# Adding the causal mask of batches 1 to 3 on GpSimd, to per-tile decay rows, instead of by a matmul into the scores

## The reference, cut to what matters

```python
def _attn_ref(q, k, v, f) -> np.ndarray:
    scores = scale * np.matmul(q, k.transpose(0, 1, 3, 2))
    log_f = np.log(np.clip(f, 0.0001, 1.0))
    cum = np.cumsum(log_f, axis=-1)
    decay = cum[:, :, :, None] - cum[:, :, None, :]
    causal = np.triu(np.ones((S, S), dtype=bool), k=1)
    scores = np.where(causal, -1000000000.0, scores + decay)
    scores = scores - np.max(scores, axis=-1, keepdims=True)
    attn = np.exp(scores)
    attn = attn / (np.sum(attn, axis=-1, keepdims=True) + 1e-09)
    return np.matmul(attn, v).astype(np.float32)
```

## Time and profile before

| what | value |
|---|---|
| median of 3 runs | 764.41 us (762.1 to 766.06) |
| the profiled execution's own time | 765.94 us |
| its span in the profile | 764.2 us |
| TensorE busy | 717.7 us (94%) |
| VectorE busy | 444.7 us (58%) |
| ScalarE busy | 437.0 us (57%) |
| GpSimd busy | 399.3 us (52%) |
| data moved | 96.65 MB, 126 GB/s over the span |

### The profile page before, as it was taken

How to read it: one execution, slowest core, us unless ns; L and a number is a source line. 1 busy time by engine, 2 the same in 40 slices (tenths; PEclk the granted TensorE clock), 3 DMA queues, 4 the chain that set the end, 5 groups by cost and what they waited for, 6 DMA issues and landing times.

```text
span 764.2 us, 15776 instructions
## 1 busy us (share of the span) xinstructions
PE 717.7 (94%) x6027; PEld 681.0 (89%) x6027; DVE 444.7 (58%) x1255; ACT 437.0 (57%) x1031; POOL 399.3 (52%) x439
## 2 busy tenths in 40 slices
PE   3999979999999999999999999999999999998993
PEld 3888879999999999999999989999999999995562
DVE  5898957676776646675656466766542332224323
ACT  4788866575757675666576665757554344311113
POOL 4355357474747764565657564848385476520000
PEclk9999989999999999999999999999999999998897
DMA  4433323332333333333331413332214454598976
GB/s 104 106 92 106 94 65 89 87 94 81 95 94 96 95 94 81 87 105 91 100 91 51 126 28 95 94 108 67 69 43 141 135 169 163 161 401 348 357 307 247
DMA packets 90362, 96.65 MB, mean 126 GB/s; under 512 B 61296, under 2 KB 61296, under 8 KB 88240
## 3 DMA queue, kind: packets, MB, share of 16 engines
q1 hardware_dynamic: 90288, 95.66, 40.6%
HBM read 90.84 MB, written 4.79 MB: 125 GB/s over the span
## 4 chain that ended last, share of the span: by engine, by line
PE 79%; DVE 10%; ACT 7%; issue 2%; DMA 0%; POOL 0%; SPq 0%; DVEq 0%; POOLq 0%
PE mb L1204 51%; PE yb L1057 6%; PE zb L1076 6%; PE xb L1103 5%; PE mb L1256 2%; DVE prob L838 2%; PE xb L1037 2%; ACT prob L689 2%; PE yb L1295 1%; ACT xh L713 1%; DVE ptl L844 1%; PE yb L1059 1%; DVE kl L806 1%; DVE qs L802 1%; ACT qs L681 1%
## 5 line engine op out<-in xcount | busy, mean ns | idle before, releaser
L1204 PE MATMUL mb<-xh,wih 128*128 128x288 f32 x512 | 159.1, 311 | 7.8 <-DVE xl L855 4.3
L1204 PE MATMUL mb<-gh,woh 128*128 128x288 f32 x512 | 156.5, 306 | 3.5 <-DVE x2t L932 3.5
L1204 PE MATMUL mb<-xl,wih 128*128 128x288 f32 x512 | 151.6, 296 | 0.0
L1204 PE MATMUL mb<-xh,wil 128*128 128x288 f32 x512 | 151.6, 296 | 0.0
L1204 PE MATMUL mb<-gl,woh 128*128 128x288 f32 x512 | 150.8, 294 | 0.0
L1204 PE MATMUL mb<-gh,wol 128*128 128x288 f32 x512 | 150.8, 294 | 0.0
L643 POOL TENSOR_TENSOR gl<-hid,gh 128x288 fp32r<-128x288 f32 x128 | 105.0, 825 | 74.9 <-ACT gh L730 73.3
L925 DVE SCALAR_TENSOR_TENSOR hid<-gate,mb 128x288 f32<-128x288 f32 x128 | 57.7, 451 | 116.0 <-ACT gate L736 114.9
L689 ACT ACTIVATE prob<-prob,m_row 64x576 f32<-64x576 f32 (+4 forms) x160 | 96.4, 604 | 35.3 <-DVE m_row L824 34.4
L660 POOL TENSOR_TENSOR wol<-stage,woh 128x512 fp32r<-128x512 f32 x64 | 82.9, 1295 | 62.0 <-ACT woh L675 62.0
L660 POOL TENSOR_TENSOR wil<-stage,wih 128x512 fp32r<-128x512 f32 x64 | 82.1, 1290 | 57.0 <-ACT wih L675 56.9
(11 more groups left out here) (196 smaller groups left out, 1471.1 us busy)
## 6 DMA issues: line engine op xcount, KB each, us to landing
stage<-in_moe_w_in SPq DMA_DIRECT2D x64, 256.0 KB, 3.0
stage<-in_moe_w_out SPq DMA_DIRECT2D x64, 256.0 KB, 2.6
ring_a<-in_moe_w SPq DMA_DIRECT2D x16, 1024.0 KB, 6.9
ring_b<-in_moe_w SPq DMA_DIRECT2D x14, 1024.0 KB, 11.8
cum_b<-cum_dram SPq DMA_DIRECT2D x32, 288.0 KB, 3.7
qk_in<-in_q SPq DMA_DIRECT2D x32, 144.0 KB, 3.0
qk_in<-in_k SPq DMA_DIRECT2D x32, 144.0 KB, 3.5
v_in<-in_v SPq DMA_DIRECT2D x32, 128.0 KB, 3.2
```

The lines of the kernel that those rows point to most:

```text
L1204: ins = mm(bank[:, 0:HALF], a[:, t, P * (j % 4):P * (j % 4) + P], x[:, t, cols], start=(i == 0), stop=(i == 11))
```

## The change

For batches 1 to 3 the mask matmul is left out. The decay row is no longer one row of 576 columns for all tiles, but one piece for each tile, `cum_t[parity]`, at the columns `COFF[i]`: tile 3 at 0, tile 0 at 512, tile 2 at 640, tile 1 at 1024 and tile 4 at 1280, 1856 columns in all. For odd heads it lies in the enlarged `cum_1`, for even heads in the part of `x2tok` that belongs to batch 2. SP loads tile 4's piece where it loaded the row before, and the other four behind the slot's loads of v, q and k. GpSimd adds the mask to the diagonal blocks of these pieces: tile 4's in a step `cmask_4` right behind dup (64x64), the others in a step `cmask` at the place of the next head's first score group near the slot's end, in two additions of two blocks each (tiles 3 and 2, then tiles 0 and 1). VectorE waits for these instead of for the load. Batch 0 stays as it was.

```diff
@@ -40,6 +40,8 @@
 QW = [128, 128, 128, 128, 64]
 POFF = [0, 128, 384, 768, 1280]
 PW = 1920
+CW = 1856
+COFF = [512, 1024, 640, 0, 1280]
 PT_ALL = 1600
 KOFF = [0, 576, 1024, 1344, 1536]
 QK_AT = 224
@@ -186,7 +188,8 @@
         dup = following_head("dup")
         early = following_head("score")
         if engine == "pool":
-            qk, dup = qk + dup, []
+            qk, dup = qk + dup + following_head("cmask_4"), []
+            early = following_head("cmask")
         norm = at(scoring, "norm", s)
         vsplit = at(scoring and engine == "pool", "vsplit", s)
         pv_first, pv = at(before, "pv_first", s - 1), at(before, "pv", s - 1)
@@ -290,7 +293,9 @@
         mask_r = sb("mask_r", [P, P], F32R, att_mem)
         qk_in = sb("qk_in", [LD, 2, NLD, 2, DIM], F32, att_mem)
         v_in = sb("v_in", [P, 2, QT, DIM], F32, att_mem)
-        cum_b = sb("cum_b", [P, 2, SEQ], F32, att_mem)
+        cum_1 = sb("cum_1", [P, CW], F32, att_mem)
+        cum_b = cum_1[:, 0:2 * SEQ].rearrange("p (x n) -> p x n", x=2)
+        cum_t = (x2tok[:, 2 * QT:3 * QT, :].rearrange("p i n -> p (i n)")[:, 0:CW], cum_1[:, :])
         qs = sb("qs", [P, 2, QT * P], F32R, att_mem)
         kh = sb("kh", [P, 2, SEQ], F32R, att_mem)
         kl = sb("kl", [P, 2, SEQ], F32R, att_mem)
@@ -370,6 +375,9 @@
         qk_dma = [sem(f"qk_dma{i}") for i in range(2)]
         v_dma = [sem(f"v_dma{i}") for i in range(2)]
         c_dma = [sem(f"c_dma{i}") for i in range(2)]
+        c_dma_4 = [sem(f"c_dma_4{i}") for i in range(2)]
+        c_masked = sem("c_masked")
+        c_masked_4 = sem("c_masked_4")
         w_dma = [sem(f"w_dma{i}") for i in range(2)]
         e_dma = [sem(f"e_dma{i}") for i in range(NR)]
         out_dma = sem("out_dma")
@@ -462,6 +470,10 @@
                 return last_tokens[i] if kind == "token" else yb[:, 0, :] if kind == "logits" else zb[:, 0, :]
             return mb[:, place[kind, m, i] % 2, :]
 
+        def cum_loaded(n):
+
+            return 16 * (n // 2 + 1) if n < HEADS else 64 + 16 * (QT - 1) * (n // 2 - 3)
+
         def is_last(m):
             return isinstance(m, int) and m == BATCH - 1
 
@@ -526,8 +538,20 @@
             def load_cum(b, s):
                 n = b * 8 + s
                 wait_from(sp, decayed, 5 * (n - 1))
-                src = cum_dram[bass.ds(n, 1), :].to_broadcast([P, SEQ])
-                sp.dma_start(cum_b[:, s % 2, :], src).then_inc(c_dma[s % 2], 16)
+                if n < HEADS:
+                    sp.dma_start(cum_b[:, s % 2, :], cum_dram[bass.ds(n, 1), :].to_broadcast([P, SEQ])
+                                 ).then_inc(c_dma[s % 2], 16)
+                    return
+                sp.dma_start(cum_t[s % 2][0:QW[4], COFF[4]:CW], cum_dram[bass.ds(n, 1), :].to_broadcast([QW[4], SEQ])
+                             ).then_inc(c_dma_4[s % 2], 16)
+
+            def load_cum_tiles(b, s):
+
+                n = b * 8 + s
+                for i in (3, 2, 0, 1) if n >= HEADS else ():
+                    w = P * i + QW[i]
+                    sp.dma_start(cum_t[s % 2][:, COFF[i]:COFF[i] + w], cum_dram[bass.ds(n, 1), 0:w].to_broadcast([P, w])
+                                 ).then_inc(c_dma[s % 2], 16)
 
             def step(b, m, st):
                 if st[0] == "load":
@@ -536,6 +560,7 @@
                     n = b * HEADS + st[1]
                     if 0 < n < BATCH * HEADS - 1:
                         load_qk((n + 1) // HEADS, (n + 1) % HEADS)
+                    load_cum_tiles(b, st[1])
                 elif st[0] == "weights":
                     load_w(st[1], st[1] // 4, st[1] % 4, 0)
                 elif st[0] == "unit":
@@ -616,6 +641,20 @@
                     pool.wait_ge(k_lo, n + 1)
                     pool.tensor_tensor(kl[64:P, par, :], kl[0:64, par, :].bitcast(F32), zero, ALU.add).then_inc(k_dup, 1)
                     pool.wait_ge(k_dup, 2 * n + 2)
+                elif st[0] == "cmask_4":
+                    n = b * 8 + st[1]
+                    if n >= HEADS:
+                        pool.wait_ge(c_dma_4[n % 2], 16 * (n // 2 - 3))
+                        at = cum_t[n % 2][0:QW[4], COFF[4] + 4 * P:CW]
+                        pool.tensor_tensor(at, at, mask[0:QW[4], 0:QW[4]], ALU.add).then_inc(c_masked_4, 1)
+                elif st[0] == "cmask":
+                    n = b * 8 + st[1]
+                    if n >= HEADS:
+                        pool.wait_ge(c_dma[n % 2], cum_loaded(n))
+                        blocks = cum_t[n % 2][:, P * 3:P * 10].rearrange("p (x n) -> p x n", n=P)
+                        for at in (blocks[:, 0:5:4, :], blocks[:, 1:7:5, :]):
+                            pool.tensor_tensor(at, at, mask[:, :].unsqueeze(1).broadcast_to([P, 2, P]), ALU.add
+                                               ).then_inc(c_masked, 1)
                 elif st[0] == "vsplit":
                     s = st[1]
                     n = b * 8 + s
@@ -815,14 +854,20 @@
                     if g == 0:
                         if s == 0 and isinstance(b, int) and b == 0:
                             dve.wait_ge(cum_out, 16)
-                        dve.wait_ge(c_dma[par], b * 64 + 16 * (s // 2 + 1))
+                        if b:
+                            dve.wait_ge(c_masked_4, b * 8 + s - HEADS + 1)
+                        else:
+                            dve.wait_ge(c_dma[par], cum_loaded(s))
                         wait_from(dve, p_tr, b * 32 + 4 * (s - 1))
+                    elif g < 3 and b:
+                        dve.wait_ge(c_masked, 2 * (b * 8 + s - HEADS) + g)
                     nc.vector.memset(carrier[:, g:g + 1], 0.0)
                     for i in SCORE_ORDER[g]:
                         r, w = QW[i], P * i + QW[i]
                         base, o = SCORE_AT[i], POFF[i]
+                        decay = cum_t[par][0:r, COFF[i]:COFF[i] + w] if b else cum_b[0:r, par, 0:w]
                         nc.vector.tensor_tensor_reduce(
-                            prob[0:r, par, o:o + w], ybf[0:r, base:base + w], cum_b[0:r, par, 0:w], 1.0, 3e38,
+                            prob[0:r, par, o:o + w], ybf[0:r, base:base + w], decay, 1.0, 3e38,
                             ALU.add, ALU.min, m_row[0:r, par, i:i + 1]).then_inc(decayed, 1)
                 elif st[0] == "norm":
                     s, par = st[1], st[1] % 2
@@ -1054,10 +1099,11 @@
                         base = SCORE_AT[i]
                         for k0, kw in ((0, HALF), (HALF, HALF)) if i == 4 else ((0, w),):
                             for x, last in ((kh, False), (kl, True)):
-                                mm(ybf[:, base + k0:base + k0 + kw], qs[:, par, P * i:P * i + P],
-                                   x[:, par, k0:k0 + kw], start=not last, stop=last, skip_group_check=True)
-                        ins = mm(ybf[:, base + P * i:base + P * i + r], ident_r[:, :], mask_r[:, 0:r],
-                                 start=False, stop=True, skip_group_check=True)
+                                ins = mm(ybf[:, base + k0:base + k0 + kw], qs[:, par, P * i:P * i + P],
+                                         x[:, par, k0:k0 + kw], start=not last, stop=last, skip_group_check=True)
+                        if b == 0:
+                            ins = mm(ybf[:, base + P * i:base + P * i + r], ident_r[:, :], mask_r[:, 0:r],
+                                     start=False, stop=True, skip_group_check=True)
                     ins.then_inc(scored, 1)
                 elif st[0] == "pt":
                     s, c = st[1], st[2]
```

## The result

The changed kernel takes 775.6 us in the median (773.9 to 777.6, 4 runs) beside 763.25 for the kernel before (4 runs): a ratio of 1.015, 95% interval 1.012 to 1.018. It is slower by 12 us where 9.2 were to be gained. Its profiled execution took 773.85 us, with a span of 772.1.

The account below looks back on a forecast made before the run. TensorE was taken as the bound in batches 1 to 3. From the profiled 765.94 us, - 13.0 + 2.0 + 1.8 gave 756.7; from the runs' median, 764.4 - 9.2 gave 755.2 us, with an 8-in-10 range of 750 to 761.

Parts of the forecast that it names:

- TensorE bounds batches 1 to 3, so a matmul less is time less: In batches 1 to 3 TensorE is always busy, so each instruction removed saves time if no other engine comes late.
- 13.0 us for 120 matmuls: On TensorE in batches 1 to 3, each removed mask matmul saves one weight load's spacing, 0.108 us; range 7 to 26.
- GpSimd gets 1.9 us a head: GpSimd's three mask additions per head take 0.36 and twice 0.76 us, 45 us over 24 heads, fitting its idle time.
- Waits for weight splits 0, for masked rows 0: GpSimd's additions make neither TensorE wait for weight splits (smallest distance 2.4 us) nor VectorE for masked rows: cost 0.
- The shared work of VectorE and GpSimd, 2.0 us in the MLP stages with a bound of 8: GpSimd's additions lengthen VectorE's normalising multiplies by up to 1.5 us, nearly covered in MLP stages: 2.0 us, between 0 and 8.
- A delay costs 0.36 us, for a quarter of the heads: In the MLP stages, delayed multiplies cost TensorE 0.36 us on x2t, taken for a quarter of the heads' additions.
- rival C: VectorE becomes the bound through late multiplies; at 1.8 us a head, 43 us are added, giving 794 us; chance 0.06.
- Batch 0, 1.8 us: At batch 0's end, without cover, additions delay head 8's multiplies by 1.2 us and the xl by 0.6: 1.8 us.
- the 1.2 us for head 8's multiplies: In batch 0's slot for head 8, GpSimd's additions fall on VectorE's multiplies: 1.2 us, between 0 and 1.8.
- The 0.6 for the xl: In the slot after head 8's, additions precede GpSimd's three xl, which release the first MLP unit: 0.6 us, between 0 and 1.9.
- SP and the DMA queues, 0: Five row loads a head instead of one, 12 MB more over 24 heads, cost 0; bound 6 us.

## Why the prediction was wrong

- **TensorE bounds batches 1 to 3, so a matmul less is time less.** Right: 10.7 us came with the matmuls alone.
- **13.0 us for 120 matmuls.** The 0.11 us each is right, at all five tiles: from the first 512-column score to the second matmul of the unit behind tiles 3, 2 and 0 it took 1.49 us before (300.42 to 301.91) and takes 1.16 now (331.30 to 332.46), for tile 4 it went from 0.76 to 0.65 and for tile 1 from 0.48 to 0.37. The total was off by a sixth, 10.7 us by the medians. Of the 2.7 us for the 24 in the undisturbed stretch 0.3 are given back at three places, two of them right behind transposes, and six of the 120 lie ahead of 101 us, where their removal moved nothing (+0.70 at 85.70 and at 101.49).
- **GpSimd gets 1.9 us a head.** 0.31 and twice 0.76 us, 43 us in all: right.
- **Waits for weight splits 0, for masked rows 0.** Right. The smallest distance of a split to its phase between 124 and 550 us is 2.2 us (2.4 before).
- **The shared work of VectorE and GpSimd, 2.0 us in the MLP stages with a bound of 8.** This is the step that failed. From 101 to 563 us the changed kernel loses 7.4 us where the run without additions gains 9.9, so the term was 17.3 us. Batch 1 carries 13.8 of it. I let a delayed group grow "by up to the 1.5 us of the pair", so by the new work that it meets. But in the changed kernel an eps step or multiply is held over several instructions of GpSimd, old and new, to the end of the run: up to 5 us, and eps and multiplies together took up to 6.5 us (218.94 to 225.46) for the 1.7 that they need. The earlier trace rows did not show that. There the multiplies stand beside two wil splits up to 211.79 and then two of them run undisturbed, 0.87 us; I read that as work slowed throughout, where two multiplies each waited for the end of one split. The long holds came with the small addition at the head of a run, to which I gave no cost but its 0.36 us, and the large pair made them 1.4 us longer. The eps step was in no term at all.
- **A delay costs 0.36 us, for a quarter of the heads.** A single price for a threshold. VectorE may be late by 1.3 to 2.1 us before TensorE waits, around the 1.6 of rival C (for five heads of batch 1, from 139.95 to 218.94, the delay of eps step and multiplies less TensorE's wait behind them); the 3.07 us, 1.8 late, stood just at that threshold, and what goes beyond it counts. TensorE's waits from 105 to 550 us grew from 8.4 to 21.7 us, and only to 9.6 without the additions. Then the clock added to it. Behind three of these pauses the granted clock was 0.60 to 0.61 for 4 us, a mixture of its two levels (1.2 and 2.4 GHz), so 1.6 us lost each time (stretches of the changed kernel, columns as in the earlier trace rows):

```profile
125.60:129.60 4.00, 3.96 (x20) 3.95 (x21) 0.69 (x2) 1.15 (x5) 0.80 (x1) 0.60 0.74 169
...
204.20:208.20 4.00, 3.98 (x20) 3.96 (x21) 1.29 (x4) 1.76 (x6) 2.03 (x2) 0.61 0.86 161
...
424.90:429.00 4.10, 4.01 (x20) 4.00 (x21) 1.46 (x4) 0.00 (x0) 2.79 (x3) 0.60 0.26 71
```

  12.1 us of waits and 4.8 of clock make 16.9 of the 17.3.
- **Batch 0, 1.8 us.** It was 1.2, TensorE's wait of 5.50 us for the first MLP unit against 4.29 before. That the table has +1.79 is chance: 0.58 of it is there since 30 us. Of the parts, the 1.2 us for head 8's multiplies was 0: they took 1.27 us, as ever, for GpSimd stood for its tile rows then, which arrived later than I had them. The 0.6 for the xl was 1.2: they were held by the additions of head 9, which waited 1.74 us for their load (timeline of GpSimd and TensorE):

```profile
97.23 1.41 POOL L656 TENSOR_TENSOR cum<-cum,mask 128x256 f32<-128x256 f32 x2 [1.74 <-DMA cum<-cum_dram]
98.60 4.63 POOL L672 TENSOR_TENSOR xl<-xst,xh 128x576 fp32r<-128x576 f32 x3
...
103.28 0.61 PE L1250 MATMUL mb<-xh,wih 128*128 128x288 f32 x1 [5.50 <-POOL xl L672]
```

- **SP and the DMA queues, 0.** Nearly right: about 0.5 us.
- **Of the rivals**, C was the one: VectorE late by its multiplies. Its price of 43 us took every head for a full loss, where batch 1 carries four fifths of it; it had 0.06. The Trainium skill (SBUF — State Buffer, its points on the engine side's ports) has the lock on the shared port pair exclusive for one whole instruction. The 30 held instructions of the kernel before agree. By that rule a wait could not exceed the longest instruction of GpSimd in these runs, 1.3 us; the eps step of 4.10 us, which outlasts three of them and the pair, doesn't agree, nor do the other holds in runs that begin with the small addition.

## What to carry to other kernels

Ask of each VectorE instruction of the kind that was held here (a tensor_scalar with all operands in SBUF) what GpSimd runs beside it, instruction by instruction, and not how busy GpSimd is. Work that is "free" on an engine with 40% idle time can turn waits for one instruction into waits for a whole run, and even an addition of 0.3 us can stand at the head of such runs. Where such an instruction is on the way to the bounding engine, give it an operand in PSUM (slower alone, 1.92 against 1.27 us, and never held), or move the new work, the small pieces too. And before a shift between two traces is put down to an edit, look whether it is there ahead of the edit: here 0.58 of 1.79 us was.

## What the runs showed of the hardware

- VectorE's tensor_scalar instructions with all operands in SBUF wait for GpSimd. In the kernel before each of the 30 held got in when the GpSimd instruction that it met ended, 10 of them with the next one following without a gap. In four kernels with the additions 41 were held on to the end of GpSimd's run, all in runs that begin with the 64x64 addition (0.31 us); the eps step of 0.17 us took up to 4.98. With gaps of 0.08 us none was held over a second instruction. (In the run without additions one eps step, begun 0.04 us before an end, at 206.26, waited out the next instruction as well.)
- A reciprocal between SBUF tiles (0.19 us in every head) and the form with an operand in PSUM were never held.
- GpSimd's instructions hardly lengthen in turn: the pairs of additions of batches 1 to 3 took 1.40 to 1.74 us, whether VectorE's multiplies ran beside them or not.
- Additions of the same size that wait for no load made the kernel slower (780 against 776 us), and 17 instead of 9 instructions of VectorE were held over further ones of GpSimd.
- Pauses of TensorE of 2.4 to 3.3 us were followed three times by 4 us at a mean granted clock of 0.60 to 0.61; one of 2.87 us (at 225.87) was not.
